# Moving a second layer's weight sums, gates and block sums between GpSimd, ScalarE and VectorE in a kernel for attention and two dense layers

## The chip, the cores and the metric

One core of a Trainium2 chip runs the whole program. The metric is the device time of one execution in microseconds (us). The engines are TensorE (PE; its weight loads are PEld in the profile), VectorE (DVE), ScalarE (ACT), GpSimd (POOL) and the queue of SyncE (SP), which here issues most DMAs.

## The reference

Everything is float32. Attention is a kernel-feature (random feature) attention without a softmax; then come two dense layers.

```python
# attention: q, k, v are (4, 8, 576, 64), omega is (128, 64)
phi(x) = exp(x @ omega.T - |x|^2/2 - rowmax) / sqrt(128)      # x = q or k, times 64^-0.25
kv = phi(k).T @ v;  z = sum over tokens of phi(k)
x = (phi(q) @ kv) / (phi(q) @ z + 1e-6)                        # then (2304 tokens, 512)
# layer 1: w_in (512, 2048), w_out (2048, 512)
h = x @ w_in;  g = h * clip(h + 3, 0, 6) / 6;  x = g @ w_out
# layer 2: the same shapes
h = x @ w_in2;  g = h * sigmoid(1.702 * h);    y = g @ w_out2
```

## The kernel before

**Precision.** Every product of the dense layers is made of three matmuls of the type fp32r: each operand is split into a high part (a rounded copy, made on ACT) and a low part (the value less its high part, a subtraction on DVE or POOL), and PE adds high x high, low x high and high x low in PSUM.

**Attention** works on 16 pairs of heads. Pairs 0 to 4 come first; pairs 5 to 15 are woven into layer 1. Time there is counted in units n of layer 1 (0 to 79) and in half-units g = 2n, 2n+1; a pair takes 8 half-units, 4 units, by the table `UNITS`. In its third half-unit `cross` (DVE, two 32x32 block transposes, L1564 and L1566) makes `q_blocks`; 16 small DMAs (`moves`, L604 on SP and L1231 on ACT) carry the blocks into `q_phi`; then ACT and DVE split it (`high_features` L1236, `low_features` L1570) and PE makes the quotient from it (`numerator`, L988).

**Layer 1** runs over 5 chunks of tokens (four of 512, the last of 256) and J = 16 feature blocks in each, so n = 0 to 79. For each n PE makes `hidden(n)` (12 matmuls into one PSUM bank `hid`), then `output(n-1)` (12 matmuls into `acc`). Between them lie `gate(n)` on ACT (L1283, h to the tile R), `gated_block(n)` on DVE (L1662), `high(n)` on ACT (L1289) and `low(n)` on DVE (L1667). There is one bank for h (two for n < 3) and one R.

**Layer 2** is a seven-product scheme of Strassen's kind: three groups c of 768 tokens, and in each a hidden stage (4 groups q of feature blocks, with 7 products each) and an output stage (7 products p, each over 4 q). A unit is one product: 12 matmuls of 384 columns (L1063 to L1065). The scheme multiplies sums of blocks, so it needs

- sums of the weights ("preps", u = 0 to 31): SP loads a raw block of 256 KB (`load_raw`, L642); POOL makes four 128x128 sums (`prepare`, L782 to L787); ACT makes two high parts (`high_combos`, L1310 and L1312); POOL makes two low parts (L790, L792); SP stores four results to the DRAM tensor `combos` (`store_combos`, L648 to L652), 896 KB in all. Preps 0 to 9 run beside attention at n = 14, 16, ..., 32 and share one buffer in `X`; the others run from n = 49 to 76 in three buffers. A load waits until the last store from its buffer has landed.
- a ring of 10 slots for weights of 512 KB (`load_combos`, L664), loaded by SP: slot by slot as the units before are done.
- sums of blocks of x (`x_first_sums`, `x_second_sum`, `x_fourth_sum`, on POOL) and of the gated blocks G (`third_and_second_sums` L831 and L833, `fourth_sum` L838, on POOL; `first_sum` L1729 on DVE), with high parts on ACT (L1334, L1354) and low parts on DVE (L1688, L1692).
- the results of the products, taken out of PSUM by DVE in the order of `TAKEN` (u2, 11, u3, 22, 21, 12; L1699 to L1713). `room` (PE) makes a product wait until its bank is free: product 24, the sixth of a group, waits for the take u3, and 43, the seventh, for the take 22.
- the gates: ACT makes the sigmoid (L1376) and POOL multiplies three of a group's four blocks by it (`gate_in_place`, L827); the take of 11 multiplies the fourth.

The last chunk of layer 1 comes out with tokens in rows. DVE turns its 32x32 blocks (L1734) and SP moves them with 32 DMAs (L696); only the third group of layer 2 reads these tokens.

The order on every engine is that of the code. Each engine works in its own order, and a wait at its head holds all behind it.

## Time and profile before

| | us |
|---|---|
| median of 3 runs (971.9 to 975.14) | 974.08 |
| the profiled execution, its own time | 973.57 |
| span of the profiled execution | 971.8 |
| PE busy | 892.7 (92%) |
| DVE busy | 552.6 (57%) |
| ACT busy | 428.6 (44%) |
| POOL busy | 433.8 (45%) |

The span goes from the first to the last instruction of the program. PE's busy time counts a pipelined matmul to its modelled end, so 92% doesn't say how near PE is to its rate; the idle stretches and the granted clock say more.

### The profile page before, as it was taken

What the parts mean: (1) busy time and instruction counts of PE and PEld (TensorE: products, weight loads), DVE (VectorE), ACT (ScalarE), POOL (GpSimd) and SP (SyncE); (2) the same over time, 40 slices, a digit from 0 to 9 for tenths busy, and PEclk for the clock granted to TensorE, in tenths of its full rate; (3) what the DMA queues carried; (4) which work ended last, traced back from release to release, by engine and by line L of the source; (5) the groups of instructions that cost most, each with busy time, mean ns of one, the idle gap of its engine ahead of it and who ended that gap; (6) DMA issues with size and microseconds to landing.
All of it is one profiled execution on the core that took longest, in us unless ns stands there. A gap on an engine that the chain in (4) does not pass through costs nothing.

```text
span 971.8 us, 13881 instructions
## 1 busy us (share of the span) xinstructions
PE 892.7 (92%) x5029; PEld 800.7 (82%) x5029; DVE 552.6 (57%) x815; ACT 428.6 (44%) x874; POOL 433.8 (45%) x428
## 2 busy tenths in 40 slices
PE   8999999678596889999999989499899998999998
PEld 8988886567475668888888879399899998999998
DVE  7876677337263566565223346247854478645673
ACT  6866755344343445454344444034343343423432
POOL 3676554334144242002777772267603676036630
...
GB/s 281 161 126 150 150 95 66 165 98 87 152 58 156 85 88 85 62 25 71 208 215 211 310 254 30 181 317 249 198 276 291 253 255 187 277 290 251 255 263 88
DMA packets 186324, 170.54 MB, mean 175 GB/s; under 512 B 87824, under 2 KB 148368, under 8 KB 186256
## 3 DMA queue, kind: packets, MB, share of 16 engines
...
## 4 chain that ended last, share of the span: by engine, by line
PE 66%; DVE 11%; SPq 7%; DMA 6%; POOL 4%; issue 3%; ACT 2%; ACTq 0%; DVEq 0%; POOLq 0%
PE acc L1063 8%; PE acc L1064 8%; PE acc L1065 8%; PE hid L1028 5%; PE hid L1029 5%; PE hid L1006 5%; PE acc L1121 4%; PE acc L1129 4%; PE acc L1128 4%; SPq L604 4%; PE att L1063 2%; PE att L1064 2%; PE att L1065 2%; DVE g L1692 2%; SPq L696 2%
## 5 line engine op out<-in xcount | busy, mean ns | idle before, releaser
L1662 DVE SCALAR_TENSOR_TENSOR R<-R,hid 128x512 f32<-128x512 f32 (+1 forms) x79 | 49.9, 631 | 170.8 <-ACT R L1283 170.8
L827 POOL TENSOR_TENSOR G<-G,gate 128x768 f32<-128x768 f32 x36 | 66.6, 1850 | 138.8 <-ACT gate L1376 138.8
L1028 PE MATMUL hid<-x_hi,w_in_hi 128*128 128x512 f32 (+1 forms) x316 | 123.7, 391 | 5.0 <-DVE R L1662 5.0
L1006 PE MATMUL hid<-x_lo,w_in_hi 128*128 128x512 f32 (+1 forms) x316 | 120.3, 381 | 0.3 <-DVE x_lo L1655 0.3
L1029 PE MATMUL hid<-x_hi,w_in_lo 128*128 128x512 f32 (+1 forms) x316 | 120.0, 380 | 0.0
L1692 DVE TENSOR_TENSOR g<-G,g 128x768 fp32r<-128x768 f32 x72 | 99.8, 1404 | 20.5 <-ACT g L1354 20.4
L1121 PE MATMUL acc<-g_hi,w_out_hi 128*128 128x512 f32 x256 | 101.1, 395 | 1.0 <-DVE g_lo L1667 0.9
L1283 ACT ACTIVATE R<-hid 128x512 f32<-128x512 f32 (+1 forms) x79 | 43.9, 555 | 123.9 <-PE hid L1006 110.0
L1128 PE MATMUL acc<-g_lo,w_out_hi 128*128 128x512 f32 x252 | 98.2, 390 | 0.0
L1129 PE MATMUL acc<-g_hi,w_out_lo 128*128 128x512 f32 x252 | 98.2, 390 | 0.0
L1354 ACT ACTIVATE g<-G 128x768 fp32r<-128x768 f32 x72 | 60.9, 847 | 72.0 <-PE acc L1065 35.4
L1667 DVE TENSOR_TENSOR g_lo<-R,g_hi 128x512 fp32r<-128x512 f32 (+1 forms) x80 | 59.3, 741 | 40.4 <-ACT g_hi L1289 40.3
L1063 PE MATMUL acc<-xhi,ring_hi 128*128 128x384 f32 x192 | 65.1, 339 | 13.9 <-DMA ring_hi<-combos 13.6
L1028 PEld LDWEIGHTS hid<-x_hi,w_in_hi 128*128 128x128 f32 x316 | 62.5, 198 | 18.7 <-DVE R L1662 7.0
L1006 PEld LDWEIGHTS hid<-x_lo,w_in_hi 128*128 128x128 f32 x316 | 62.0, 196 | 12.4 <-DVE x_lo L1655 1.3
L1029 PEld LDWEIGHTS hid<-x_hi,w_in_lo 128*128 128x128 f32 x316 | 62.4, 198 | 9.8
L1063 PE MATMUL acc<-g,ring_hi 128*128 128x384 f32 x192 | 65.3, 340 | 5.3 <-issue 5.3
L1065 PE MATMUL acc<-g,ring_hi 128*128 128x384 f32 x192 | 65.3, 340 | 0.0
L1064 PE MATMUL acc<-g,ring_hi 128*128 128x384 f32 x192 | 65.3, 340 | 0.0
L1376 ACT ACTIVATE gate<-G 128x768 f32<-128x768 f32 x36 | 30.5, 847 | 78.8 <-DVE G L1706 65.1
L1065 PE MATMUL acc<-xlo,ring_hi 128*128 128x384 f32 x192 | 64.9, 338 | 0.0
L1064 PE MATMUL acc<-xhi,ring_hi 128*128 128x384 f32 x192 | 64.9, 338 | 0.0
...
## 6 DMA issues: line engine op xcount, KB each, us to landing
...
```

The lines of the kernel that those rows point to most:

```text
L827: nc.gpsimd.tensor_tensor(g, g, R2[:, k % 2], ALU.mult).then_inc(gated2, 1)
L1006: return nc.tensor.matmul(hid_bank(n)[:, 0:t], w_hi[0][:, s * 512 + k * P:s * 512 + (k + 1) * P], x_lo[:, k, x0:x0 + t], start=False, stop ...
L1028: nc.tensor.matmul(bank, w_hi[0][:, at], x_hi[:, k, x0:x0 + t], start=(k == 0), stop=False)
L1029: nc.tensor.matmul(bank, w_lo[0][:, at], x_hi[:, k, x0:x0 + t], start=False, stop=False)
L1063: nc.tensor.matmul(to, w[:, at:at + P], high[:, k, :], start=opens and k == 0, stop=False, skip_group_check=True)
L1064: nc.tensor.matmul(to, w[:, at + P:at + 2 * P], high[:, k, :], start=False, stop=False, skip_group_check=True)
L1065: last = nc.tensor.matmul(to, w[:, at:at + P], low[:, k, :], start=False, stop=closes and k == 1, skip_group_check=True)
L1121: nc.tensor.matmul(bank, w_hi[1][:, at], g_hi[:, g, 0:t], start=(s == 0), stop=False)
L1128: nc.tensor.matmul(bank, w_hi[1][:, at], g_lo[:, g, 0:t], start=False, stop=False)
L1129: last = nc.tensor.matmul(bank, w_lo[1][:, at], g_hi[:, g, 0:t], start=False, stop=(s == J - 1))
L1354: nc.scalar.activation(g2[q][:, 0], feature(q, p), ACT.Copy).then_inc(g2_high, 1)
L1692: nc.vector.tensor_tensor(g2[q][:, 1], feature(q, p), g2[q][:, 0].bitcast(F32), ALU.subtract).then_inc(g2_ready, 1)
```

## The change

The weight sums are scheduled in half-units (`prep_half`). Eight instead of ten run beside attention, and all of their arithmetic is on POOL; the other 24 have sums on POOL, high parts on ACT, low parts on DVE, four buffers instead of three, and run 20 from half-unit 96 on at one in 1.6 half-units, and 4 more in the last chunk. From n = 49 on h alternates between two PSUM banks and R between two tiles, so that `hidden(n)` and `gate(n)` wait for the block before the last. In layer 2 the gates, the second, third and fourth sums and the sums of x for groups 1 and 2 are DVE's; POOL keeps those of x for group 0 (the first pair of them 8 units earlier). The 32 row moves are issued one by one between ring loads 28 to 59.

```diff
...
-EARLY_PREP = 10
+EARLY_PREP = 8
+LAST_PREP = 28
...
+    TWO_BANKS = 3 * J + 1
...
-        late = [at_place(f"stage{i}", [P, 1920], stage_base + i * 1920 * 4) for i in range(3)]
+        late = [at_place(f"stage{i}", [P, 1920], at) for i, at in
+                enumerate([stage_base, stage_base + 7680, stage_base + 15360, cols_base])]
+        R_odd = at_place("R_odd", [P, CH_MAX], cols_base + 7680)
 
...
         def hid_bank(n):
-            return att[0] if n == 1 else hid
+            return att[0] if n == 1 else att2 if n >= TWO_BANKS and n % 2 else hid
+
+        def gates_before(n):
+
+            return n - 1 if n >= TWO_BANKS else n
...
         def R_of(n):
-            return R[:, 0:size(n)]
+            return (R_odd if n >= TWO_BANKS and n % 2 else R)[:, 0:size(n)]
...
-        def prep_step(u):
-
-            if u < EARLY_PREP:
-                return 14 + 2 * u
+        def prep_half(u):
+
             v = u - EARLY_PREP
-            return 49 + v if v < 15 else 64 + 2 * (v - 15)
-
-        def load_step(u):
-            return prep_step(u) - (1 if u < EARLY_PREP else 2)
-
-        def preps_at(n, step):
-            return [u for u in range(PREPS) if step(u) == n]
+            return 26 + 4 * u if v < 0 else 6 * J + v * 8 // 5 if u < LAST_PREP else 8 * J + 4 * (u - LAST_PREP)
+
+        def preps_at(half, early, late_by):
+
+            return [u for u in range(PREPS) if half == prep_half(u) + (early if u < EARLY_PREP else late_by + 2 * (u >= LAST_PREP and late_by > 2))]
 
         def stage_of(u):
 
-            return 3 if u < EARLY_PREP else (u - EARLY_PREP) % 3
+            return (u - EARLY_PREP) % 4 if u >= EARLY_PREP else 4
 
         def uses_of(u):
 
-            return u + 1 if u < EARLY_PREP else (u - EARLY_PREP) // 3 + 1
+            return u + 1 if u < EARLY_PREP else (u - EARLY_PREP) // 4 + 1
 
...
+                for u in preps_at(g, 4, 4):
+                    store_combos(u)
+                for u in preps_at(g, 0, 0):
+                    load_raw(u)
                 if g % 2 == 0:
-                    for u in preps_at(g // 2 - 1, prep_step):
-                        store_combos(u)
-                    for u in preps_at(g // 2, load_step):
...
-            for tile in range(2):
-                sp.wait_ge(rows_turned, tile + 1)
-                for i in range(4):
-                    for j in range(4):
-                        sp.dma_start(*row_move(tile, i, j)).then_inc(rows_moved[tile], 16)
+            row_moves = {A_UNITS + k: (k // 16, k // 4 % 4, k % 4) for k in range(32)}
...
                 if i < SUPERS * UNITS2:
                     load_combos(i)
+                if i in row_moves:
+                    tile, *of_tile = row_moves[i]
+                    sp.wait_ge(rows_turned, tile + 1)
+                    sp.dma_start(*row_move(tile, *of_tile)).then_inc(rows_moved[tile], 16)
...
+            def early_combos(u):
+                raw, sums_u, high, sums_high = stage(u)
+                nc.gpsimd.tensor_copy(high, raw[:, 0:3 * P]).then_inc(prep_high, 1)
                 pool.wait_ge(prep_added, 4 * u + 4)
+                nc.gpsimd.tensor_copy(sums_high, sums_u).then_inc(prep_high, 1)
+
+            def early_lows(u):
+                raw, sums_u, high, sums_high = stage(u)
                 pool.wait_ge(prep_high, 2 * u + 1)
                 nc.gpsimd.tensor_tensor(raw[:, 0:3 * P].bitcast(F32R), raw[:, 0:3 * P], high.bitcast(F32), ALU.subtract).then_inc(prep_low, 1)
                 pool.wait_ge(prep_high, 2 * u + 2)
                 nc.gpsimd.tensor_tensor(sums_u.bitcast(F32R), sums_u, sums_high.bitcast(F32), ALU.subtract).then_inc(prep_low, 1)
...
+                for u in preps_at(g, 2, 2):
+                    prepare(u)
+                    if u < EARLY_PREP:
+                        early_combos(u)
+                        early_lows(u)
+                if g == 2 * (LAST1 + 3):
+                    x_first_sums()
+            x_second_sum()
+            x_fourth_sum()
...
-                    pe.wait_ge(gated, n)
+                    if n == TWO_BANKS:
+                        pe.wait_ge(den_ready, dens_to(PAIRS - 1, 1, 1))
+                    pe.wait_ge(gated, gates_before(n))
...
+            def late_highs(half):
+                for u in preps_at(half, 3, 3):
+                    if u >= EARLY_PREP:
+                        high_combos(u)
...
+                late_highs(2 * n)
                 if not keys:
                     high(n)
+                late_highs(2 * n + 1)
...
-                for u in preps_at(n, prep_step):
-                    high_combos(u)
...
+            def low_combos(u):
+                raw, sums_u, high, sums_high = stage(u)
+                dve.wait_ge(prep_high, 2 * u + 1)
+                dve.wait_ge(prep_added, 4 * u + 4)
+                nc.vector.tensor_tensor(raw[:, 0:3 * P].bitcast(F32R), raw[:, 0:3 * P], high.bitcast(F32), ALU.subtract).then_inc(prep_low, 1)
+                dve.wait_ge(prep_high, 2 * u + 2)
+                nc.vector.tensor_tensor(sums_u.bitcast(F32R), sums_u, sums_high.bitcast(F32), ALU.subtract).then_inc(prep_low, 1)
+
+            def late_lows(half):
+                for u in preps_at(half, 3, 3):
+                    if u >= EARLY_PREP:
+                        low_combos(u)
...
+            def gate_in_place(c, q, what):
+
+                k = 4 * (c * GROUPS2 + q) + ("11", "22", "21", "12").index(what)
+                dve.wait_ge(sig_ready, k + 1)
+                dve.wait_ge(taken, taken_to(hidden_group(c, q), what))
+                g = hidden_part(c, q, what)
+                nc.vector.tensor_tensor(g, g, R2[:, k % 2], ALU.mult).then_inc(gated2, 1)
...
+            def third_sum(c, q):
+                dve.wait_ge(t1_ready, c * GROUPS2 + q + 1)
+                nc.vector.tensor_tensor(of_pairs(G12, q), of_pairs(G22, q), of_pairs(G12, q), ALU.subtract).then_inc(t3_ready, 1)
+
+            def second_sum(c, q):
+                dve.wait_ge(t1_ready, c * GROUPS2 + q + 1)
+                dve.wait_ge(g2_ready, g2_entry(c, 0, q))
+                nc.vector.tensor_tensor(of_pairs(G11, q), of_pairs(G22, q), T1_of(q), ALU.subtract).then_inc(t2_ready, 1)
+
+            def fourth_sum(c, q):
+                dve.wait_ge(g2_ready, g2_entry(c, 2, q))
+                dve.wait_ge(t2_ready, c * GROUPS2 + q + 1)
+                nc.vector.tensor_tensor(of_pairs(G21, q), of_pairs(G21, q), of_pairs(G11, q), ALU.subtract).then_inc(t4_ready, 1)
...
+            def x_first_sums(c):
+
+                dve.wait_ge(unit_done, hidden_unit(c - 1, GROUPS2 - 1, 6) + 1)
+                if c == SUPERS - 1:
+                    for moved_tile in rows_moved:
+                        dve.wait_ge(moved_tile, 256)
+                dve.wait_ge(evac_act, 2 * CHUNKS)
+                dve.wait_ge(evac_dve, 2 * CHUNKS)
+                b11, b12, b22 = x_block(c, 0, 0), x_block(c, 0, 1), x_block(c, 1, 1)
+                nc.vector.tensor_tensor(x_sum, in_quarters(b12), in_quarters(b11), ALU.subtract).then_inc(x_added, 1)
+                dve.wait_ge(x_added, 4 * c + 1)
+                nc.vector.tensor_tensor(b12, b22, b12, ALU.subtract).then_inc(x_added, 1)
+
+            def x_second_sum(c):
+                dve.wait_ge(x_added, 4 * c + 2)
+                dve.wait_ge(xc_ready, 7 * c + 1)
+                nc.vector.tensor_tensor(in_quarters(x_block(c, 0, 0)), in_quarters(x_block(c, 1, 1)), x_sum, ALU.subtract).then_inc(x_added, 1)
+
+            def x_fourth_sum(c):
+                dve.wait_ge(xc_ready, 7 * c + 3)
+                dve.wait_ge(x_added, 4 * c + 3)
+                nc.vector.tensor_tensor(x_block(c, 1, 0), x_block(c, 1, 0), x_block(c, 0, 0), ALU.subtract).then_inc(x_added, 1)
...
+                late_lows(2 * n)
                 low(n)
+                late_lows(2 * n + 1)
...
                     take_hidden(c, q, "u2")
                     if first:
                         x_low(0, 4)
-                    if q > 0:
-                        first_sum(c, q - 1)
+                    else:
+                        if q > 0:
+                            gate_in_place(c, q - 1, "12")
+                            first_sum(c, q - 1)
                     take_hidden(c, q, "11")
                     if first:
                         x_low(0, 5)
                         x_low(0, 6)
+                    elif q > 0:
+                        third_sum(c, q - 1)
                     take_hidden(c, q, "u3")
                     if first:
                         for tile in range(2):
                             turned_rows(tile)
-                    else:
+                    elif q > 0:
+                        second_sum(c, q - 1)
+                    take_hidden(c, q, "22")
+                    if not first:
                         g2_low_part(c, 0, q)
-                    take_hidden(c, q, "22")
                     take_hidden(c, q, "21")
+                    gate_in_place(c, q, "22")
                     if first:
                         g2_low_part(c, 0, q)
                     take_hidden(c, q, "12")
-                first_sum(c, GROUPS2 - 1)
+                    gate_in_place(c, q, "21")
+                last = GROUPS2 - 1
+                gate_in_place(c, last, "12")
+                first_sum(c, last)
+                second_sum(c, last)
+                third_sum(c, last)
                 for p in range(1, len(PRODUCTS)):
                     for q in range(GROUPS2):
-                        if p > 1 and q == GROUPS2 - 1:
+                        if p > 1 and q == last:
                             take_output(c, TAKEN[p - 2])
                         g2_low_part(c, p, q)
+                        if p == 1 and q == 1 and c + 1 < SUPERS:
+                            x_first_sums(c + 1)
+                        elif p in (3, 4) and q < 2:
+                            fourth_sum(c, q + 2 * (p - 3))
                     if c + 1 < SUPERS:
                         x_low(c + 1, p - 1)
-                        if p == len(PRODUCTS) - 1:
+                        if p == 1:
+                            x_second_sum(c + 1)
+                        elif p == 4:
+                            x_fourth_sum(c + 1)
```

ScalarE, beside attention at the end of n = 16 and into n = 17 (X<-X are the high parts of prep 1, R<-hid is `gate(17)`, q_hi<-q_phi the high parts of the queries). Before:

```order
L1231 DMA q_phi<-q_blocks 32x9x32
L1220 ACTIVATE k_phi<-att,bias 128x128 x8
L1299 ACTIVATE X<-acc 128x512 x2
L1231 DMA q_phi<-q_blocks 32x9x32 x5
L1310 ACTIVATE X<-X 128x384
L1312 ACTIVATE X<-X 128x512
L1283 ACTIVATE R<-hid 128x512
L1236 ACTIVATE q_hi<-q_phi 128x576
```

ScalarE at the same place in the changed kernel:

```order
L1207 DMA q_phi<-q_blocks 32x9x32
L1196 ACTIVATE k_phi<-att,bias 128x128 x8
L1276 ACTIVATE X<-acc 128x512 x2
L1207 DMA q_phi<-q_blocks 32x9x32 x5
L1259 ACTIVATE R<-hid 128x512
L1212 ACTIVATE q_hi<-q_phi 128x576
```

The two high parts of the prep are gone from ScalarE; they stand on GpSimd as two casts behind the prep's sums.

SyncE's queue, where layer 2 begins (ring slots are loads of weights, X<-q_cols and X<-k_cols the row moves). Before:

```order
L664 DMA ring_hi<-combos 128x1024 x2
L696 DMA X<-q_cols 32x4x32 x16
L696 DMA X<-k_cols 32x4x32 x16
L664 DMA ring_hi<-combos 128x1024
L664 DMA ring_lo<-combos 128x1024
```

The same stretch of SyncE's queue in the changed kernel:

```order
L669 DMA ring_hi<-combos 128x1024 x7
L669 DMA ring_lo<-combos 128x1024
L669 DMA ring_hi<-combos 128x1024
L669 DMA ring_lo<-combos 128x1024
L669 DMA ring_hi<-combos 128x1024 x5
L707 DMA X<-q_cols 32x4x32
L669 DMA ring_hi<-combos 128x1024
L707 DMA X<-q_cols 32x4x32
L669 DMA ring_hi<-combos 128x1024
```

The 32 row moves stood in one piece ahead of the eleventh ring load; now the first of them stands behind ring load 28 and the others follow one at a time.

VectorE, one group of layer 2's hidden stage (c = 0, q = 3; G11 to G22 are the four gated blocks, T1 the first sum, gate2 the sigmoid, g2_3 the parts of q = 3). Before:

```order
L1699 TENSOR_TENSOR G12_58<-acc23,G21_59 128x768
L1729 TENSOR_TENSOR T1_high_62<-G12_58,G11_57 128x768
L1713 TENSOR_TENSOR G11_57<-att01,gate2_78 128x768
L1701 TENSOR_TENSOR G22_60<-acc23,G21_59 128x768
L1692 TENSOR_TENSOR g2_3_82<-G11_57,g2_3_82 128x768
L1706 TENSOR_TENSOR G22_60<-acc01,G22_60 128x768
L1703 TENSOR_TENSOR G21_59<-acc23,G21_59 128x768
L1706 TENSOR_TENSOR G12_58<-acc01,G12_58 128x768
```

VectorE, the same group in the changed kernel, from the take of u2 to the take of 12:

```order
L1695 TENSOR_TENSOR G12_58<-acc23,G21_59 128x768
L1727 TENSOR_TENSOR G12_58<-G12_58,gate2_78 128x768
L1733 TENSOR_TENSOR T1_high_62<-G12_58,G11_57 128x768
L1709 TENSOR_TENSOR G11_57<-att01,gate2_78 128x768
L1737 TENSOR_TENSOR G12_58<-G22_60,G12_58 128x768
L1697 TENSOR_TENSOR G22_60<-acc23,G21_59 128x768
L1742 TENSOR_TENSOR G11_57<-G22_60,T1_high_62 128x768
L1702 TENSOR_TENSOR G22_60<-acc01,G22_60 128x768
L1688 TENSOR_TENSOR g2_3_82<-G11_57,g2_3_82 128x768
L1699 TENSOR_TENSOR G21_59<-acc23,G21_59 128x768
L1727 TENSOR_TENSOR G22_60<-G22_60,gate2_78 128x768
L1702 TENSOR_TENSOR G12_58<-acc01,G12_58 128x768
```

Between the takes now stand two gates and the third and second sums, and one more gate follows the last row: 13 instructions a group in place of 8.

## Rows read from the trace of the kernel before

**Rows 1.** The page: its span.

```profile
span 971.8 us, 13881 instructions
```

**Rows 2.** Windows: us, busy of PE, PEld, DVE, ACT, POOL, clock, DMA share, GB/s.

```profile
163.20:366.00 202.80, 158.46 (x813) 128.72 (x814) 103.44 (x180) 83.18 (x207) 70.38 (x94) 0.88 0.44 109
366.00:422.80 56.80, 56.80 (x324) 47.53 (x323) 36.70 (x65) 27.99 (x73) 6.61 (x8) 1.00 0.31 64
448.00:530.00 82.00, 82.00 (x363) 67.85 (x363) 21.90 (x32) 32.84 (x61) 55.57 (x84) 1.00 0.65 184
530.00:588.00 58.00, 53.40 (x318) 47.38 (x317) 24.22 (x42) 27.45 (x61) 37.57 (x49) 0.97 0.86 265
664.00:694.00 30.00, 26.80 (x149) 25.26 (x148) 26.57 (x15) 14.12 (x18) 26.31 (x12) 1.00 0.80 238
694.00:787.00 93.00, 93.00 (x529) 93.00 (x528) 51.48 (x55) 32.34 (x39) 32.21 (x18) 0.98 0.81 259
```

**Rows 3.** Timeline of ACT: start, duration, what, [idle before, what ended it].

```profile
163.21 0.60 ACT L1283 ACTIVATE R<-hid 128x512 f32<-128x512 f32 x1
...
178.10 0.52 ACT L1310 ACTIVATE X<-X 128x384 fp32r<-128x384 f32 x1 [8.00 <-DMA X<-w_raw]
...
365.99 0.60 ACT L1283 ACTIVATE R<-hid 128x512 f32<-128x512 f32 x1 [4.43 <-PE hid L1006]
...
422.77 0.60 ACT L1283 ACTIVATE R<-hid 128x512 f32<-128x512 f32 x1 [4.16 <-PE hid L1006]
```

**Rows 4.** Timeline of SP's queue: issues after one pair's transposes.

```profile
164.49 5.59 SPq L604 DMA_DIRECT2D q_phi<-q_blocks  x8
...
171.91 0.82 SPq L652 DMA_DIRECT2D combos<-X  x1
175.46 0.35 SPq L642 DMA_DIRECT2D X<-w_raw  x1
...
188.29 0.58 SPq L581 DMA_DIRECT2D rows<-k_n  x1
```

**Rows 5.** Waits: engine, line <- releaser: us in total, times, longest.

```profile
PE att L988 <- DVE state_lo L1549: 42.3, 5, 9.3
...
ACT X L1310 <- DMA X<-w_raw: 40.1, 5, 8.9
...
PE acc L1063 <- DMA ring_hi<-combos: 13.6, 1, 13.6
```

**Rows 6.** Timeline of POOL: one prep, then the squares of one row tile.

```profile
178.15 0.46 POOL L782 TENSOR_TENSOR X<-X 128x128 f32<-128x128 f32 x1 [17.59 <-DMA X<-w_raw]
...
181.00 1.27 POOL L792 TENSOR_TENSOR X<-X 128x512 fp32r<-128x512 f32 x1
188.89 1.15 POOL L736 TENSOR_TENSOR rows<-rows 128x576 f32<-128x576 f32 x1 [6.62 <-DMA rows<-q_n]
...
191.78 0.82 POOL L742 TENSOR_TENSOR rows<-rows 128x144 f32<-128x144 f32 x1
```

**Rows 7.** Groups of POOL by form: xcount | busy us, mean ns | idle before.

```profile
L756 POOL CAST w_out_hi<-X 128x512 fp32r<-128x512 f32 x3 | 1.9, 617 | 0.0
```

**Rows 8.** Timeline of PE in the last chunk of layer 1.

```profile
578.59 0.58 PE L1028 MATMUL hid<-x_hi,w_in_hi 128*128 128x256 f32 x1 [2.67 <-DVE R L1662]
```

**Rows 9.** Timeline of SP's queue at the start of layer 2.

```profile
598.77 10.89 SPq L696 DMA_DIRECT2D X<-q_cols  x16
...
620.00 0.59 SPq L664 DMA_DIRECT2D ring_hi<-combos  x1
```

**Rows 10.** Windows (columns as in rows 2): the 40 us behind that wait.

```profile
624.00:664.00 40.00, 39.94 (x215) 39.97 (x216) 19.30 (x20) 11.54 (x14) 20.18 (x11) 0.93 0.88 322
```

**Rows 11.** Timeline of DVE where layer 2 passes to its output stage.

```profile
669.11 6.00 DVE L1692 TENSOR_TENSOR g<-G,g 128x768 fp32r<-128x768 f32 x3
...
677.56 2.59 DVE L1688 TENSOR_TENSOR xlo<-X,xhi 128x768 fp32r<-128x768 f32 x1
```

**Rows 12.** Windows (columns as in rows 2): one group of the hidden stage.

```profile
641.55:656.12 14.57, 14.57 (x86) 14.57 (x85) 7.78 (x8) 5.02 (x7) 9.23 (x6) 1.00 0.77 258
```

83 lines of the change are left out of this document (21 added, 62 removed).

## The prediction

> **What bounds the kernel now.** I read the page first, then windows over its stages, then the chain of waits and, at each place where PE stands idle, the timeline of the engine that it waits for. The profiled execution took 973.57 us, its span is 971.8 [rows 1], and the median of the three runs shown is 974.08, so sums are made against 973.6 and need 0.5 more for the median. PE's busy share is no guide, so the windows are read for idle time and for the granted clock.
>
> In windows [rows 2], PE is never idle and its clock full from 366 to 422.8 and from 448 to 530, and from 694 on there are 93 us without a gap. There the kernel runs at PE's rate, and nothing that other engines save can shorten it. Time is lost in four places.
>
> First, 163.2 to 366: PE is busy for 158.5 of 202.8 us at a clock of 0.88. The gates of n = 16 and n = 36 are its ends, five pairs of heads; the gates of n = 36 and n = 44 are 56.8 us apart, two pairs [rows 3]. So a pair takes 28.4 us where no weight sums run and 40.6 where they do. The chain of waits shows what happens once a pair: SP issues the block moves (8 in 5.6 us), then the stores of a prep, waits until the last has landed (171.91 to 175.46), and only then loads the next raw block [rows 4]. ACT stands in `high_combos` for that block: 8.00 us idle, until 178.10 [rows 3]. Behind it in ACT's order are `gate(17)` and `high_features`, and PE waits for what follows them: five waits of 42.3 us in all for `state_lo`, as many as ACT's waits for `X<-w_raw` (40.1) [rows 5]. `state_lo` itself is only queued on DVE behind `gated_block`, which waits for that gate. The other 20 us of the 60.8 are PE's lower clock behind each gap, and ACT's waits for POOL's sums.
>
> Second, the last chunk: 53.4 busy of 58.0 us, clock 0.97 [rows 2], with one wait of 2.67 for DVE's R [rows 8]. Third, the start of layer 2: SP issues 32 row moves from 598.77 to 620.00, the eleventh ring load stands behind them [rows 9], and PE waits 13.6 us for it [rows 5]. Fourth, the passage to the output stage of groups 0 and 1: 3.2 us idle (664 to 694), then a clock of 0.98 over 93 us, 1.9 more [rows 2]. There DVE and POOL work against each other: three low parts take 6.00 us and one takes 2.59 [rows 11], while in the hidden stage eight DVE instructions take 7.78, 0.97 each [rows 12].
>
> **The change part by part.**
>
> *Preps beside attention.* ACT's two high parts go, and with them its wait for the load. The moves, the splits and the quotient then follow as in the pairs without preps: 202.8 - 5 x 28.4 = 60.8 us at most. What comes in its place is on POOL and SP. A prep on POOL took 178.15 to 182.27, 4.1 us, for sums and lows [rows 6]; two casts of 384 and 512 columns join it, at 0.62 for 512 [rows 7] about 1.1, so 5.2. SP is queued behind POOL now: its stores wait for POOL's casts and lows, and behind them stand the next load, the columns, rows and values of the next pair and its moves. One round of two preps is a loop: store landed 3.5, raw block landed 2.6 [rows 4, 3], prep 5.2, last stores issued 0.9, landed 3.5, row tile loaded about 3 (as the raw block, a bit more), its squares 3.7 (188.89 to 192.60 [rows 6]), the second prep 5.2, stores issued 0.9: 28.5 us, against 28.4 of a pair. The seven us of moves lie beside the squares and the second prep. SP was through with its round 24 us after the transposes (164.49 to 188.87 [rows 4]), and POOL's casts add some 2 to that. So the loop just fits. DVE's `norms` behind the transposes needs the squares at about the moment they are done. I charge 1 us for each of four pairs for that and 2 for the two chunk changes that lie in this stretch and not in the free pairs: gain 60.8 - 6 = **54.8**. The lower end of this cost is 0; the upper, with each of the loop's landings 1 us later (4.5 a round), is 18.
>
> *Preps 8 to 27 in n = 48 to 63.* PE is covered now, so nothing can be won; the second bank for h wins nothing either where PE has no gap. One prep comes every 1.6 half-units of 2.72 us, 4.35 us, in place of 5.44. POOL needs 1.8 of them. ACT has 1.2 and DVE about 1.3 for a prep, by the width of the row for 768 columns, beside their own work of a unit; in this stretch now they are busy 32.8 and 21.9 of 82 us [rows 2], so both have idle time for it. What is near its limit is the DMA: a prep moves 1.18 MB, 271 GB/s at this pace; the share was 0.65 at 184 GB/s [rows 2], so some 0.96. Cover is the four buffers: a load goes out more than three half-units (8 us) before ACT wants it. Cost taken: **1**, from 0 to 10 (half a us for each of 20 preps).
>
> *Last chunk.* Loss now: 4.6 idle and 0.03 x 58 = 1.7 of clock. Four preps instead of about a dozen, the loads earlier, and two banks and two R give ACT and DVE a unit's slack. The first sums of x still meet DVE's lows there. Gain **4.3** of the 6.3.
>
> *Row moves.* They go between loads 28 to 59, while the ring is ten units ahead (some 20 us); a move costs SP 0.65 us (21.2 us for 32 [rows 9]) of the 2.08 of a unit, and a load some 0.5. The wait of 13.6 goes, and the clock behind it (0.93 over 40 us [rows 10]: 2.8); DVE is fuller in this first group, for which I take 0.5 off: gain **15.9**. Only group 2 needs the moved rows, some 25 units after the last of them.
>
> *Gates and sums on DVE.* A hidden group lasts 14.57 us on PE, and DVE goes from 8 to 13 instructions. At 0.97 [rows 12] that is 12.6 us: it fits. The order matters more than the sum: let PE finish product 12, the group's third, at 0. Take 11 follows the sigmoid (ACT's seven instructions of a group take 5.02 [rows 12], a long one some 0.9), 0.9 to 1.9, then the third sum to 2.8, the take u3 to 3.8, and PE asks for u3 at 4.2 (two units); the second sum to 4.7, the take 22 to 5.7, wanted at 6.2. The margins are 0.4 to 0.5 us. At the passage, the last gate, three sums and the first lows end about 7 us after the hidden stage; PE wants the first at 8.3. With POOL idle nothing slows the lows: 2 x (3.2 + 1.9) = 10.2, gain **10.2**.
>
> The Trainium skill speaks against such a move: Perfetto Trace Analysis, section Optimizing Scalar/DVE Operations, says that GpSimd and VectorE share an SBUF read port, so that offloading between the two might not help; SBUF, section Who interferes with whom, adds that a VectorE instruction with two SBUF inputs and a GpSimd one that reads SBUF exclude each other, the later one waiting for the whole of the first. The trace agrees with the second: 2.59 for a low part beside POOL's sums, 0.97 without [rows 11, 12]. By the first, the gain of 10.2 would be 0 and the time 899.6. By the second it comes back whole, because no GpSimd work is left there.
>
> Sum: 54.8 - 1 + 4.3 + 15.9 + 10.2 = 84.2, and 973.6 - 84.2 = **889.4 us**.
>
> **Rivals.**
>
> *The loop of SP and POOL sets attention's pace.* For it: 28.5 against 28.4, four DMA landings in series, SP in order. Against: the loop's terms are measured in a loaded stretch, and only four pairs are concerned. Price 18 in place of 4: 903 us.
>
> *The late preps starve ACT.* For it: a DMA share of 0.96, and DVE's lows meeting POOL's sums of 0.46 each [rows 6]. Against: four buffers, POOL at less than half. Price 10 in place of 1, and PE's first gaps there would lower its clock: 898 to 902.
>
> *ACT's wait is not what holds the pair.* If the moves and SP's queue behind them held it, the gap would stay in half: 27 less is won, 916. Against it, `q_phi` was complete long before 178 us, and the pairs without preps have the same moves.
>
> *The passages keep their loss.* DVE gets three sums and a gate there ahead of the first low part, 3.9 us of its own; if that does what POOL's contention did, the 10.2 stay lost: 900. Against it, 7 us of work stand against 8.3.
>
> *VectorE becomes the bound of layer 2, slower than before.* If the seven instructions of a group that read two SBUF operands (low, three sums, three gates) cost what they do at the passage, 2.59, a group takes 6 x 0.97 + 7 x 2.59 = 23.9 us on DVE against 14.57 on PE; 12 groups x 9.4 = 113 us, the time 889 + 113 = 1002. It decides from 2.3 us an instruction. Against it, nothing else runs on POOL there.
>
> **How the numbers follow.** Forecast 0.60 (its own range 879 to 896); the loop 0.17; the late preps 0.11; ACT's wait not the cause 0.06; the passages 0.02; VectorE the bound 0.02; no measurable change 0.01; 0.01 for other losses. From both ends: all costs at 0 give 973.6 - 60.8 - 6.3 - 16.4 - 10.2 = 880, and a few us less if attention's pairs get below 28.4; costs of 18 and 5 give 907. The range is 877 to 908; it holds the forecast, the first two rivals and the passages but for their edges, some 0.85. A change under 0.3% (3 us) can't be told from none here: faster 0.97, within it 0.01, slower 0.02.
>
> **What would show it.** Gates of n = 16 and n = 36 some 148 us apart, no wait of ACT for `X<-w_raw`, PE's clock at 1.00 in that stretch. No wait of PE for the ring at the start of layer 2. Low parts at 0.96 in the output stages, POOL idle, DVE near 85% in hidden stages and PE without gaps of a us. PE's windows over n = 48 to 63 still full. I am wrong where POOL or SP hold DVE's `norms` or the moves (gates more than 30 us apart by pair), where PE waits for `g_lo` in n = 48 to 63, or where it waits for the takes u3 and 22 in each group.

## The result and the profile after

The changed kernel takes 889.73 us (median of 4 runs, 887.95 to 890.35) against 974.61 for the kernel before beside it (4 runs): a ratio of 0.9131, 95% interval 0.9108 to 0.9153. The forecast was 889.4. The profiled execution took 890.09, its span is 888.3, so 83.5 of span are gone; the sum of the prediction had 84.2.

The page of the changed kernel, its span, PE's row and the clock in 40 slices, first:

```profile
span 888.3 us, 13924 instructions
...
PE 871.9 (98%) x5029; PEld 787.7 (89%) x5029; DVE 616.6 (69%) x943; ACT 418.4 (47%) x858; POOL 233.0 (26%) x316
...
PEclk9999999999999999999999999999999999999999
```

Where the time came from is read with two kinds of view. ACT's timeline gives the start of `gate(n)`, at which the program is cut into stretches; these two stand for the rows of before in [rows 3], and the third is gate 64:

```profile
163.13 0.60 ACT L1259 ACTIVATE R<-hid 128x512 f32<-128x512 f32 x1 [0.34 <-DVE g_lo L1649]
...
313.46 0.60 ACT L1259 ACTIVATE R<-hid 128x512 f32<-128x512 f32 x1 [4.13 <-PE hid L980]
...
481.49 0.38 ACT L1259 ACTIVATE R<-hid 128x256 f32<-128x256 f32 x1
```

The windows, with the columns of [rows 2], show what is left idle in each. In order: attention beside layer 1; two pairs without weight sums; 15 units with late preps; the last chunk; its first unit; one of its units further on; the hidden stage at the start of layer 2; one group of it (third of c = 0); its passage to the first output stage; and the 93 us behind that. Layer 2 runs 70 us earlier than before, so the last two are the stages of 664:694 and 694:787 in [rows 2].

```profile
163.13:313.46 150.33, 146.19 (x812) 120.29 (x813) 103.70 (x180) 73.95 (x189) 71.81 (x96) 0.99 0.54 132
313.46:370.49 57.03, 57.03 (x325) 47.70 (x325) 35.63 (x65) 27.89 (x72) 6.71 (x8) 1.00 0.31 63
395.75:477.35 81.60, 81.60 (x361) 67.57 (x360) 43.78 (x66) 34.51 (x67) 37.77 (x73) 1.00 0.82 242
481.49:531.39 49.90, 46.01 (x277) 41.21 (x278) 27.91 (x48) 19.14 (x46) 13.46 (x20) 0.97 0.79 242
481.49:487.28 5.79, 4.45 (x24) 3.75 (x24) 5.31 (x10) 2.71 (x7) 0.10 (x1) 1.00 1.04 297
503.57:508.83 5.26, 4.66 (x19) 4.08 (x20) 2.38 (x5) 1.71 (x5) 1.32 (x3) 0.68 1.01 294
550.00:594.00 44.00, 44.00 (x255) 43.85 (x254) 36.74 (x41) 14.95 (x18) 0.00 (x0) 1.00 0.79 250
568.20:582.77 14.57, 14.57 (x86) 14.57 (x85) 11.72 (x13) 5.02 (x6) 0.00 (x0) 1.00 0.80 251
594.00:624.00 30.00, 30.00 (x175) 30.00 (x174) 27.25 (x31) 15.52 (x19) 0.00 (x0) 1.00 0.87 264
624.00:717.00 93.00, 93.00 (x539) 93.00 (x538) 67.34 (x75) 34.05 (x41) 0.00 (x0) 1.00 0.87 272
```

From gate 16 to gate 36 it is now 150.3 us, at a clock of 0.99; before it was 202.8 at 0.88 [rows 2]. The units with late preps are full. Layer 2 has no idle time of PE in any of its windows, and POOL none of its work; the chain of waits has one wait of PE in it, 0.3 us. The only loss of size is in the last chunk: 3.9 us idle and a clock of 0.97, nearly what it was.

The chain of waits lists little more for PE than these, and for DVE one that is new. They stand where [rows 5] had 42.3, 40.1 and 13.6:

```profile
DVE half_norm L1481 <- POOL rows L747: 7.8, 3, 3.8
...
PE acc L1097 <- DVE g_lo L1649: 4.0, 3, 1.4
...
PE hid L1004 <- DVE R L1644: 2.4, 2, 1.5
...
PE acc L1014 <- DVE g_lo L1649: 2.2, 1, 2.2
```

The length of each stretch, as the difference of two starts of `gate(n)` in ACT's timeline (the last one runs to the end of the span), gives the balance by term for every kernel below. All later sections speak by its columns.

| kernel | to gate 16 | 16 to 36 | 36 to 64 | 64 to 79 | 79 to end | span |
|---|---|---|---|---|---|---|
| before | 163.2 | 202.8 | 167.9 | 50.8 | 387.1 | 971.8 |
| changed | 163.1 | 150.3 | 168.0 | 49.9 | 356.9 | 888.3 |
| before + casts on POOL | 162.9 | 163.5 | 168.1 | 51.0 | 387.4 | 932.9 |
| before + row moves spread | 163.3 | 204.3 | 167.9 | 50.8 | 370.6 | 956.8 |
| before + layer 2 on DVE | 163.3 | 204.1 | 167.9 | 51.0 | 374.7 | 961.0 |
| changed, casts back on ACT | 163.0 | 188.9 | 168.0 | 49.0 | 356.9 | 925.8 |
| changed, ten early preps | 162.9 | 162.5 | 168.1 | 45.0 | 356.9 | 895.4 |
| changed, one bank | 162.7 | 150.3 | 169.5 | 49.6 | 356.9 | 889.0 |
| changed, x opening on DVE | 163.3 | 150.1 | 168.1 | 45.9 | 356.9 | 884.3 |
| changed, row load ahead | 161.6 | 147.6 | 168.1 | 47.9 | 356.9 | 882.1 |
| changed, both of these | 161.6 | 146.8 | 168.1 | 46.1 | 356.9 | 879.6 |
| changed, two more a group | 164.4 | 150.3 | 168.1 | 49.8 | 361.5 | 894.0 |

The stretch to gate 16 moves by up to 1.7 us between kernels that have the same orders there, so differences of a single column below about that size are not read as effects. In the kernel with one bank `gate(64)` on ACT starts 2.97 us behind PE's first matmul of the last chunk (482.52 and 479.55), where it starts 1.62 behind in the changed kernel and 1.64 in the one before. Its columns 36 to 64 and 64 to 79 are shifted against the others by about 1.35 us for that reason, and are compared below from PE's matmul.

### The profile page after: what moved, and what is told of

It reads as the page before. It is cut to its first block, busy times and chain, and to the rows that moved or that the text cites. A ratio compares the mean times of both kernels' runs of the same rounds, so it can differ in the third digit from the quotient of the medians.

```text
span 888.3 us, 13924 instructions
## 1 busy us (share of the span) xinstructions
PE 871.9 (98%) x5029; PEld 787.7 (89%) x5029; DVE 616.6 (69%) x943; ACT 418.4 (47%) x858; POOL 233.0 (26%) x316
## 4 chain that ended last, share of the span: by engine, by line
PE 83%; DVE 6%; DMA 4%; SPq 3%; POOL 2%; ACT 1%; issue 1%; ACTq 0%; DVEq 0%; POOLq 0%
PE acc L1039 9%; PE acc L1041 9%; PE acc L1040 9%; PE acc L1097 5%; PE acc L1105 5%; PE acc L1104 5%; PE hid L1004 5%; PE hid L980 4%; PE hid L1005 4%; PE att L1041 4%; PE att L1039 4%; PE att L1040 4%; PE att L919 3%; PE att L882 2%; DMA combos<-X 2%; SPq L609 1%
## 5 line engine op out<-in xcount | busy, mean ns | idle before, releaser
L1004 PE MATMUL hid<-x_hi,w_in_hi 128*128 128x512 f32 (+1 forms) x252 | 97.8, 388 | 2.4 <-DVE R L1644 2.4
L980 PE MATMUL hid<-x_lo,w_in_hi 128*128 128x512 f32 (+1 forms) x252 | 95.5, 379 | 0.6 <-DVE x_lo L1637 0.4
L1005 PE MATMUL hid<-x_hi,w_in_lo 128*128 128x512 f32 (+1 forms) x252 | 94.9, 377 | 0.0
L1688 DVE TENSOR_TENSOR g<-G,g 128x768 fp32r<-128x768 f32 x72 | 68.1, 955 | 24.9 <-ACT g L1336 24.9
L1644 DVE SCALAR_TENSOR_TENSOR R<-R,hid 128x512 f32<-128x512 f32 (+1 forms) x63 | 40.9, 649 | 57.3 <-ACT R L1259 57.2
L1649 DVE TENSOR_TENSOR g_lo<-R,g_hi 128x512 fp32r<-128x512 f32 (+1 forms) x64 | 46.5, 727 | 26.8 <-ACT g_hi L1265 26.6
L1617 DVE RECIPROCAL k_phi<-k_phi 128x288 f32<-128x288 f32 x24 | 46.8, 1949 | 20.6 <-ACT k_phi L1226 20.6
L1097 PEld LDWEIGHTS acc<-g_hi,w_out_hi 128*128 128x128 f32 x256 | 48.5, 189 | 13.9 <-DVE g_lo L1649 3.1
L1004 PEld LDWEIGHTS hid<-x_hi,w_in_hi 128*128 128x128 f32 x252 | 47.4, 188 | 13.2 <-DVE R L1644 3.3
L980 PEld LDWEIGHTS hid<-x_lo,w_in_hi 128*128 128x128 f32 x252 | 47.4, 188 | 11.1 <-DVE x_lo L1637 2.1
```

What stands on the lines that cost most here:

```text
L980: return nc.tensor.matmul(hid_bank(n)[:, 0:t], w_hi[0][:, s * 512 + k * P:s * 512 + (k + 1) * P], x_lo[:, k, x0:x0 + t], start=False, stop ...
L1004: nc.tensor.matmul(bank, w_hi[0][:, at], x_hi[:, k, x0:x0 + t], start=(k == 0), stop=False)
L1005: nc.tensor.matmul(bank, w_lo[0][:, at], x_hi[:, k, x0:x0 + t], start=False, stop=False)
L1097: nc.tensor.matmul(bank, w_hi[1][:, at], g_hi[:, g, 0:t], start=(s == 0), stop=False)
L1617: nc.vector.reciprocal(d, d).then_inc(recip_done, 1)
L1688: nc.vector.tensor_tensor(g2[q][:, 1], feature(q, p), g2[q][:, 0].bitcast(F32), ALU.subtract).then_inc(g2_ready, 1)
```

## The experiments

### One part of the change at a time, in the kernel before

**The casts alone.** The early preps' high parts go from ACT to POOL, with ten early preps and everything else as before.

```diff
                 nc.gpsimd.tensor_tensor(s4, second, s2, ALU.subtract).then_inc(prep_added, 1)
+                if u < EARLY_PREP:
+                    nc.gpsimd.tensor_copy(high, raw[:, 0:3 * P]).then_inc(prep_high, 1)
                 pool.wait_ge(prep_added, 4 * u + 4)
+                if u < EARLY_PREP:
+                    nc.gpsimd.tensor_copy(sums_high, sums_u).then_inc(prep_high, 1)
...
                 for u in preps_at(n, prep_step):
-                    high_combos(u)
+                    if u >= EARLY_PREP:
+                        high_combos(u)
```

> The kernel before with one edit: the high parts of the ten preps beside attention are made by GpSimd instead of ScalarE. If ScalarE's wait for the raw block holds each pair of heads (my theory), five stalls of some 8 us and the low clock behind them go and nearly all of the 60.8 us comes back, less about 1.5 us a pair for the fuller GpSimd: 920 to 928 us, and no wait of ScalarE for X<-w_raw. If the block moves and SyncE's queue hold the pair (rival), half stays: about 947 us. If most of the 52 us gained in this stretch came from other parts of the change (rival), it stays above 960.

Measured: 933.88 us, ratio 0.9597 (0.9579 to 0.9615). It is 6 us above the theory's range. ACT's wait for `X<-w_raw` is gone and four pairs take 28.7 to 31.0 us, near the free pace of 28.4, so the mechanism holds; but the fifth still takes 42.7 (41.4 in the kernel before). The chain of waits of this kernel shows it:

```profile
ACT X L1253 <- DMA combos<-X: 10.5, 1, 10.5
...
PE att L992 <- ACT k_phi L1254: 7.0, 1, 7.0
```

The quotient of pair 12 writes into memory that the early preps used, so ACT waits ahead of it until the last store of the last early prep has landed. With ten preps that is prep 9 at n = 32, and ACT stands for 10.5 us. In the kernel before only 2.7 us of this wait showed, at 347.27: ACT had just stood for 8.1 us for the raw block of prep 9, until 339.60, in the same pair, and so came late to the quotient too. The change removes it by running only eight preps there, the part of the diff to which the prediction gave no price.

**The row moves alone.** The 32 moves go between loads 28 to 59.

```diff
-            for tile in range(2):
-                sp.wait_ge(rows_turned, tile + 1)
-                for i in range(4):
-                    for j in range(4):
-                        sp.dma_start(*row_move(tile, i, j)).then_inc(rows_moved[tile], 16)
+            row_moves = {A_UNITS + k: (k // 16, k // 4 % 4, k % 4) for k in range(32)}
...
                 if i < SUPERS * UNITS2:
                     load_combos(i)
+                if i in row_moves:
+                    tile, *of_tile = row_moves[i]
+                    sp.wait_ge(rows_turned, tile + 1)
+                    sp.dma_start(*row_move(tile, *of_tile)).then_inc(rows_moved[tile], 16)
```

> The kernel before with one edit: the 32 row moves are issued one by one between ring loads 28 to 59. Theory: the wait of 13.6 us for the ring and 2.8 us of clock behind it go, 958 us (956 to 960), ratio 0.983. Rival: without the wait VectorE's crowded first group holds PE, and 4 us or more of the gain is lost: 962 or above.

Measured: 957.72 us, ratio 0.9847 (0.9832 to 0.9863), as expected. Layer 2 is 16.5 us shorter, PE's wait for the ring is not listed any more, and the window in which the clock had been 0.93 [rows 10] is full:

```profile
620.00:664.00 44.00, 44.00 (x256) 44.00 (x255) 27.07 (x23) 17.51 (x22) 31.71 (x16) 1.00 0.83 260
```

**Layer 2 on VectorE alone.** The gates, the sums of G and the x sums of groups 1 and 2 go from POOL to DVE, in the changed kernel's order; the row moves stay in one block. Its core (the functions and the loop are those of the change):

```diff
-            def gate_in_place(c, q, what):
-                ...
-                nc.gpsimd.tensor_tensor(...)
+            def gate_in_place(c, q, what):
+                ...
+                nc.vector.tensor_tensor(...)
```

> The kernel before with one edit: layer 2's gates, its second, third and fourth sums and the sums of x for groups 1 and 2 on VectorE. Theory: GpSimd and VectorE no longer slow each other at the two passages, 10 us gained: 964 us (962 to 966), low parts at 0.96 us instead of 1.40. Rival one, VectorE short of time in hidden groups: waits of PE for the takes u3 and 22, 0.5 us or more in each of 12 groups, and the time at 970 or above. Rival two, the part gains more than the passages: below 961, which would explain why layer 2 in the changed kernel gave 30 us where 26 were summed.

Measured: 959.87 us, ratio 0.9876 (0.9856 to 0.9896), 2 us below the theory's range and in that of rival two: the part gains more than the passages. Layer 2 is 12.4 us shorter. From the groups by line, the 72 low parts of G, in the kernel before and in this one:

```profile
L1692 DVE TENSOR_TENSOR g<-G,g 128x768 fp32r<-128x768 f32 x72 | 99.8, 1404 | 20.5 <-ACT g L1354 20.4
...
L1659 DVE TENSOR_TENSOR g<-G,g 128x768 fp32r<-128x768 f32 x72 | 68.1, 956 | 24.8 <-ACT g L1321 24.8
```

From the chain of waits, PE's wait for the ring:

```profile
PE acc L1030 <- DMA ring_hi<-combos: 15.1, 1, 15.1
```

The low parts cost what they cost alone, and the waits at the passages are gone. The ring wait is 1.5 us longer than before [rows 5], so this change wins 13.9, and SP's block of moves takes 1.5 of it back: PE came sooner to the same late load. Together with the row moves that 1.5 is free again: 16.5 + 12.4 + 1.5 = 30.4, against 30.2 in the changed kernel.

The kernel before shows which of DVE's instructions POOL slows. Three lines of one of its hidden groups, the first and the second of DVE, the third of POOL:

```profile
644.51 1.34 DVE L1692 TENSOR_TENSOR g<-G,g 128x768 fp32r<-128x768 f32 x1
...
649.88 0.96 DVE L1706 TENSOR_TENSOR G<-acc,G 128x768 f32<-128x768 f32 x1 [1.12 <-PE acc L1065]
...
649.71 1.85 POOL L827 TENSOR_TENSOR G<-G,gate 128x768 f32<-128x768 f32 x1 [0.18 <-ACT gate L1376]
```

The take at 649.88 reads PSUM and one block in SBUF, lies wholly beside a gate on POOL, and takes its usual 0.96. The low part at 644.51 reads two blocks in SBUF, begins beside a sum on POOL, and takes 1.34. So the 0.97 of [rows 12] is not a price without POOL, as the prediction has it: POOL is busy for 9.23 us of that group. Most of DVE's instructions in it are takes.

The Trainium skill (SBUF — State Buffer, section Who interferes with whom) says that a VectorE instruction with two SBUF inputs and a GpSimd one that reads SBUF contend, and that one of them waits for the whole of the other. The runs agree: 956 ns without POOL, 1,404 on average with it. The Trainium skill's caution in Perfetto Trace Analysis, section Optimizing Scalar/DVE Operations, that offloading between the two might not help, is not borne out where everything on POOL goes: 12.4 us came back.

### Attention: which part of the change won it

**The casts back.** The changed kernel, still with eight early preps, but ACT makes their high parts, at the end of its unit.

```diff
-                        early_combos(u)
...
+                for u in preps_at(2 * n, 2, 3):
+                    if u < EARLY_PREP:
+                        high_combos(u)
```

> The changed kernel, eight preps beside attention, but their high parts are on ScalarE again, at the end of its unit as before the change. All else is as changed. Theory (ScalarE's wait for the raw block, once a pair, is what costs most of attention's 52 us): the wait for X<-w_raw is back in four pairs, and n = 16 to 36 takes 185 to 195 us against 150.3: the 202.8 of before less some 12 for the two preps that are gone; the time is 924 to 934 us. Rival (it is the number of preps, or SyncE's order of issue, that held the pairs, and GpSimd's casts only rearranged work): n = 16 to 36 stays below 165 us, the time below 904.

Measured: 929.58 us, ratio 0.9554 (0.9534 to 0.9575), in the range of the theory and far from the rival's. From the chain of waits and the window from gate 16 to gate 36:

```profile
PE att L956 <- DVE state_lo L1528: 33.6, 4, 8.9
...
ACT X L1281 <- DMA X<-w_raw: 32.1, 4, 8.9
```

```profile
162.95:351.86 188.91, 154.05 (x812) 126.12 (x813) 102.49 (x180) 81.11 (x203) 61.53 (x82) 0.90 0.43 105
```

Four waits of ACT, four of PE behind them, 8 us each: 38.6 us for four pairs, 9.6 a pair. PE is idle for 30.7 of the 38.6 (34.9 against 4.1); for the other 7.9 it is busy longer on the same 812 matmuls, at a clock of 0.90 over the stretch against 0.99.

**Ten early preps.** The changed kernel with `EARLY_PREP = 10`; the waits for the last stores count on accordingly.

```diff
-EARLY_PREP = 8
+EARLY_PREP = 10
...
-                    act.wait_ge(stored_prep[3], 64 * uses_of(PREPS - 1))
+                    act.wait_ge(stored_prep[3], 64 * uses_of(PREPS - 3))
```

> The changed kernel with ten preps beside attention instead of eight (22 late ones). The run with GpSimd's casts alone kept one stall of some 8 us at n = 33 and 34. If that stall is ScalarE's wait, ahead of the quotient of pair 12, for the stores of the last early prep, it comes back here: 13 us more between the gates of n = 16 and n = 36, 901 to 904 us, with ScalarE waiting for combos<-X. Rival: the stall came from the late preps' or the low clock's side of the kernel before, and this one stays within 2 us of the changed kernel, 888 to 892.

Measured: 898.14 us, ratio 0.9231 (0.9213 to 0.9248). The stall of the first experiment is back, in one pair:

```profile
308.56 0.61 PE L962 MATMUL att<-q_hi,state_hi 128*128 128x288 f32 x1 [7.01 <-ACT k_phi L1226]
```

From 16 to 36 it costs 12.2 us, as expected. The last chunk is 4.9 us shorter, and that was not expected; the time is 3 us below the expected range for it. The late preps end two earlier there, and PE's wait for `g_lo` on the output side (2.2 us in the changed kernel) is down to 0.5, and the one at the change of chunk from 1.34 to 0.28.

So the 52.5 us of attention are two gains. Taking the casts off ACT is worth 39.3 us in the kernel before and 38.6 in the changed one; two preps fewer are worth 13.2 with the casts on POOL (163.5 to 150.3, the other way 12.2) and 13.9 with the casts on ACT (202.8 to 188.9). Either order gives the same two sizes. Over the whole program the two preps are worth less than 12 or 13 us, since the last chunk takes 4.9 of it back: the kernel with ten is 8.4 us slower by the medians.

**The row load ahead.** What is left of the loop of SP and POOL: DVE's `half_norm` waits for the squares of the row tile. SP's timeline of the changed kernel, one round, shows where its load stands:

```profile
164.41 5.61 SPq L609 DMA_DIRECT2D q_phi<-q_blocks  x8
...
181.05 0.38 SPq L653 DMA_DIRECT2D combos<-X  x1
...
187.21 0.34 SPq L647 DMA_DIRECT2D X<-w_raw  x1
187.59 0.43 SPq L586 DMA_DIRECT2D rows<-q_n  x1
...
191.01 6.95 SPq L609 DMA_DIRECT2D q_phi<-q_blocks  x10
```

`rows<-q_n` stands behind the stores of a prep and the wait for their landing. One half-unit earlier it stands ahead of them:

```diff
-                a = at_slot(g, 6)
+                a = at_slot(g, 5)
                 if a is not None and a + 2 < PAIRS:
                     rows_of(a + 2, KQ)
+                a = at_slot(g, 6)
                 if a is not None and a + 1 < PAIRS:
                     values(a + 1)
```

> The changed kernel with one DMA moved: SyncE loads the row tile of the pair after next ahead of the store and the load of the odd prep, not behind them. Theory: the loop of SyncE and GpSimd is as long as a pair, and VectorE's wait for GpSimd's squares (7.8 us in 3) is its only cost; it goes, and with it two gaps of PE of 0.9 and 1.5 us: 887 to 888.5 us. Rival, the loop costs nothing that counts: same time within 0.5 us. Rival, the loop was nearer to being the pace than I think: 885 or less.

Measured: 885.17 us, ratio 0.9096 (0.9078 to 0.9114), 1.8 us below the theory's range and just above the rival's 885. `half_norm` no longer waits, and 16 to 36 is 2.7 us shorter, which is about what was expected of this part. Another 3.5 us are in two other columns. The 1.5 ahead of gate 16 may be the edit's, which moves the same load for pairs before n = 16 too: both kernels with it have 161.6 there. The 2.0 in the last chunk are left unexplained.

### The last chunk

**One bank, one R.** The changed kernel with `hid` alone, in the whole of layer 1.

```diff
-    TWO_BANKS = 3 * J + 1
+    TWO_BANKS = 10 * J
```

> The changed kernel with one edit: h stays in one PSUM bank and R in one tile to the end of layer 1. Theory: nothing in the 16 units of the fourth chunk, where PE has no gap now, if the preps' 2.4 us on ScalarE and VectorE fit behind a single bank; in the last chunk, where ScalarE and VectorE fall behind twice, 1 to 3 us more: 890 to 893. Rival: the closer preps of the fourth chunk need the second bank, and each of 20 preps costs 0.5 us or more: 900 or above, with waits of PE for R from n = 49 to 63.

Measured: 890.57 us, ratio 0.9158 (0.9139 to 0.9177); by the time it is not told apart from the changed kernel. The two columns of the balance mislead here: `gate(64)` waits for `g_lo`, since with one R it must. PE's first matmul of the last chunk is the better mark. In the kernel with one bank, then in the changed one:

```profile
479.55 0.28 PE L1004 MATMUL hid<-x_hi,w_in_hi 128*128 128x256 f32 x1
...
482.52 0.38 ACT L1259 ACTIVATE R<-hid 128x256 f32<-128x256 f32 x1 [1.29 <-DVE g_lo L1649]
...
479.87 0.28 PE L1004 MATMUL hid<-x_hi,w_in_hi 128*128 128x256 f32 x1
```

From gate 36 to this matmul the two take 166.5 and 166.4 us, so one bank costs nothing in the fourth chunk. From the matmul to gate 79 they take 52.55 and 51.52: the second bank and the second R are worth 1.0 us in the last chunk, at the low end of the theory's 1 to 3. Each figure is read from one execution, so a difference of this size is a reading and no proof.

**The opening sums of x on VectorE.** The timeline of the changed kernel where PE stands longest in this chunk:

```profile
498.37 1.85 POOL L813 TENSOR_TENSOR x_sum<-X 128x768 f32<-128x768 f32 x1
498.52 2.12 DVE L1669 TENSOR_TENSOR stage<-stage 128x384 fp32r<-128x384 f32 x1 [0.43 <-POOL stage L792]
...
500.31 2.03 POOL L815 TENSOR_TENSOR X<-X 128x768 f32<-128x768 f32 x1
500.56 2.31 DVE L1671 TENSOR_TENSOR stage<-stage 128x512 fp32r<-128x512 f32 x1
...
504.17 0.80 PE L1014 MATMUL acc<-w_out_hi,g_hi 128*128 128x512 f32 x1 [2.23 <-DVE g_lo L1649]
...
505.35 0.56 DVE L1669 TENSOR_TENSOR stage<-stage 128x384 fp32r<-128x384 f32 x1
505.87 0.69 DVE L1671 TENSOR_TENSOR stage<-stage 128x512 fp32r<-128x512 f32 x1
```

Two low parts of a prep take 2.12 and 2.31 us beside POOL's two sums of x, and 0.56 and 0.69 seven us later without them. That is 3.2 us more on DVE in units of 2.8, PE waits 2.23, and the clock of the unit around it is 0.68 (window above). The experiment gives the two sums to DVE, behind its work for n = 73 and 74.

```diff
+            def x_opening(i):
+
+                b11, b12, b22 = x_block(0, 0, 0), x_block(0, 0, 1), x_block(0, 1, 1)
+                if i == 0:
+                    ...
+                    nc.vector.tensor_tensor(x_sum, in_quarters(b12), in_quarters(b11), ALU.subtract).then_inc(x_added, 1)
+                else:
+                    dve.wait_ge(x_added, 1)
+                    nc.vector.tensor_tensor(b12, b22, b12, ALU.subtract).then_inc(x_added, 1)
...
+                if n - LAST1 - 9 in (0, 1):
+                    x_opening(n - LAST1 - 9)
```

> The changed kernel with the first two sums of x for group 0 on VectorE, behind the low parts of n = 73 and 74, instead of GpSimd at n = 67. If the loss of 4 us at n = 69 to 71 is VectorE's two low parts standing 2.12 and 2.31 us beside those sums (0.55 and 0.69 elsewhere), it goes: 885 to 887 us, no PE gap of 2 us near 504. Rival: the place is short of ScalarE's or the DMA's time, and 1 us or less comes back.

Measured: 886.45 us, ratio 0.911 (0.9093 to 0.9127), as expected. The gap is gone and the last chunk takes 45.9 us, 4.0 less. On DVE the first of the sums takes 0.95 us, on POOL it took 1.85, and the low parts are short again:

```profile
504.30 0.56 DVE L1658 TENSOR_TENSOR stage<-stage 128x384 fp32r<-128x384 f32 x1 [0.42 <-POOL stage L792]
504.90 0.69 DVE L1660 TENSOR_TENSOR stage<-stage 128x512 fp32r<-128x512 f32 x1
...
512.24 0.95 DVE L1669 TENSOR_TENSOR x_sum<-X 128x768 f32<-128x768 f32 x1
```

The edit moves the sums to another engine and some six units later at once, so it shows what their meeting with the low parts cost, and not that VectorE is the better engine for them.

**Both.** The row load ahead and the opening sums on DVE, as above.

> The changed kernel with both repairs: VectorE makes the first two sums of x for group 0, and SyncE loads the row tile of q and k one half-unit earlier. They act at different places. From the segments of the two runs: attention (n = 16 to 36) 147.6 as with the row load alone, the last chunk (n = 64 to 79) 44 to 46 us against 49.9, everything else as in the changed kernel. Theory (the two losses are independent): 880 to 883.5 us. Rival: part of what the earlier row load gained (2 us in the last chunk) is the same loss that the sums of x made, or was chance; then the last chunk stays at 45.9 and attention near 150, and the time is 884 to 886.

Measured: 881.61 us (5 runs, 881.37 to 882.77), ratio 0.9071 (0.9053 to 0.9089), as the theory had it. This interval lies below that of the changed kernel (0.9108 to 0.9153), which those of the two single edits do not: it is the fastest version here. The last chunk gains no more than with the sums alone, so the 2 us that the row load seemed to win there were not an addition to them.

### Layer 2: how near DVE is to its limit

**Two more instructions a group.** In the four hidden groups of c = 2, DVE gets two instructions (768 and 640 columns, their results unused) between the third sum and the take u3.

```diff
                     elif q > 0:
                         third_sum(c, q - 1)
+                    if c == SUPERS - 1:
+                        for pad, wide in zip(pads, (384, 320)):
+                            x = x_block(0, 0, 0)[:, :, 0:wide]
+                            nc.vector.tensor_tensor(pad, x, x, ALU.max)
```

> The changed kernel with two idle instructions more on VectorE (768 and 640 columns, read from finished blocks, written to scratch) ahead of the take u3 in each of the four hidden groups of c = 2. VectorE has then 14.4 us of work in a group of 14.57. If the order's margin of 0.4 us before u3 is what counts, PE waits 1 to 1.5 us a group, 4 to 6 us in all: 894 to 896. If only the sum counts, nothing is lost: 889 to 891.

Measured: 893.7 us, ratio 0.9179 (0.9155 to 0.9204), 0.3 us below the theory's range; layer 2 takes 4.6 us more, and the rival that only the sum counts falls. DVE's 13 instructions are busy for 11.72 of a group's 14.57 us, so 1.6 more would still fit. The timeline shows that they don't fit where they stand:

```profile
792.93 0.95 DVE L1898 TENSOR_TENSOR pad_a<-X 128x768 f32<-128x768 f32 x1
...
793.80 0.82 DVE L1898 TENSOR_TENSOR pad_b<-X 128x640 f32<-128x640 f32 x1
...
794.54 0.95 DVE L1698 TENSOR_TENSOR G<-acc,G 128x768 f32<-128x768 f32 x1
...
794.14 0.34 PE L1042 MATMUL acc<-xlo,ring_lo 128*128 128x384 f32 x1
795.54 0.44 PE L1040 MATMUL acc<-xhi,ring_hi 128*128 128x384 f32 x1 [1.07 <-DVE G L1698]
```

The take u3 is pushed back by 794.54 - 792.93 = 1.61 us. PE's matmuls start every 0.17 us here, so after the one at 794.14 the product that needs the bank would have started at 794.31; it starts 1.23 late (the 1.07 in the row counts from the end of the matmul before). So its margin was 1.61 - 1.23 = 0.38 us, where the prediction had 0.4. The second to fourth group have this wait of 1.07; the first, in which no gate or third sum precedes the take, has 0.20.

## Why the prediction was right

**Attention beside the preps** (54.8 forecast, 52.5 measured). What bounded it was read rightly: with the casts back on ACT, four waits return and with them 38.6 us. The loop was sized nearly right: SP's moves of the six pairs begin at 164.41, 191.01, 221.43, 249.79, 285.13 and 310.75, 25.6 to 35.3 apart and 29.3 on average, against 28.5 for the loop. POOL's prep takes 5.6 us (178.05 to 183.67, from the rows below) against 5.2, and the time lost against the free pace is 150.3 - 5 x 28.5 = 7.8 against the 6 charged. Of that, the row load ahead takes 2.7 away; the other 5 are not assigned. POOL's timeline, one prep with its casts:

```profile
178.05 0.46 POOL L787 TENSOR_TENSOR X<-X 128x128 f32<-128x128 f32 x1 [15.57 <-DMA X<-w_raw]
...
179.96 0.50 POOL L796 CAST X<-X 128x384 fp32r<-128x384 f32 x1
180.41 0.62 POOL L798 CAST X<-X 128x512 fp32r<-128x512 f32 x1
...
181.95 1.72 POOL L805 TENSOR_TENSOR X<-X 128x512 fp32r<-128x512 f32 x1
```

Wrong in one step: "ACT's two high parts go, and with them its wait for the load. The moves, the splits and the quotient then follow as in the pairs without preps." In the fifth pair they don't, as long as there are ten preps; ACT then waits for a store. The prediction took the gap of each of the five pairs to be of one kind and ascribed all to the casts. About a quarter of the gain, 13 us, belongs to the move of two preps out of this stretch. The number was right because the change does both. For the casts alone the same working, with 1 us for each of five pairs and 2 for the chunk changes, gives 60.8 - 7 = 53.8 us; the first experiment measured 39.3. The loop as a rival (903) and the wait as no cause (916) both fall.

**Late preps** (1 forecast, nothing measured). PE is full from n = 49 to 63, at a DMA share of 0.82 and 242 GB/s where 0.96 had been estimated. The 0.1 more in 36 to 64 is below what can be read.

**Last chunk** (4.3 forecast, 0.9 measured). This term was mis-sized. "Two banks and two R give ACT and DVE a unit's slack" is worth 1.0 us by the kernel with one bank. "The first sums of x still meet DVE's lows there" was named, but only the 2.0 us that the prediction left of the 6.3 could stand for it; it costs 4.0 with its clock, as the opening sums on DVE show. Without it the chunk gains 50.8 - 45.9 = 4.9, near the 4.3 of the forecast. Part of what remains is at the change of chunk (PE waits in the window 481.49 to 487.28), where the splits of x and the lows of preps both stand on DVE. With ten early preps, whose late preps end sooner, PE's wait there is 0.28 us instead of 1.34; no experiment was made for this place alone.

**Row moves** (15.9 forecast, 16.5 measured alone). Right in mechanism and size.

**Gates and sums on DVE** (10.2 forecast; 12.4 alone, 13.9 with the time that the ring wait took back). The mechanism was right, though the 0.97 "without" was read in a group where POOL is at work; with POOL idle the low parts take 0.956. The size was 3.7 too small. Of that, 1.3 us are a wait of PE for ACT's `G` (L1361) at the start of layer 2, listed in the trace of before and, with 1.3 again, in that of the row moves alone, but not in this kernel's; the prediction overlooked it. The other 2.4 us stay unassigned. Where VectorE could have become the bound, it did not: no instruction of the group nears the 2.3 us from which it would decide, and DVE is busy for 80% of a hidden group, 85% forecast.

The errors have both signs: attention 2.3 and the last chunk 3.4 less than forecast, late preps 0.9 and layer 2 4.1 more. The nearness of 889.4 to 889.7 owes something to that.
